# Expert layer in pieces of 64 rows: two experts per step on the two column halves of TensorE

## The reference

```
logits = einsum('bsd,de->bse', x, w_gate)
local_gate = sigmoid(x @ w_local)
for b, for s:
    fresh_e = argmax(logits[b, s])
    e = fresh_e if s == 0 or local_gate[b, s] < 0.5 else prev_e
    prev_e = e
    p = softmax(logits[b, s])
    h = maximum(x[b, s] @ w1[e], 0)
    out[b, s] = p[e] * (h @ w2[e])
```

## Time and profile before

| | |
|---|---|
| median of 3 runs | 992.5 us (991.58 to 993.65) |
| the profiled execution | 993.9 us, of it 992.2 us span |
| TensorE matmuls busy | 947.2 us (95%) |
| TensorE weight loads busy | 732.5 us (74%) |
| VectorE busy | 465.9 us (47%) |
| ScalarE busy | 270.5 us (27%) |
| GpSimd busy | 275.8 us (28%) |
| first matmul of the expert stage | 686.3 us |

### The profile page before, as it was taken

The page is one execution under the profiler, slowest core; times in us unless marked ns, Lnnn a source line. Parts: engine busy times, 40 slices in busy tenths (PEclk is TensorE's granted clock), DMA queues, the critical chain, the costliest instruction groups (busy, mean ns, idle before and its releaser), DMA issues.

```text
span 992.2 us, 51897 instructions
## 1 busy us (share of the span) xinstructions
PE 947.2 (95%) x23581; PEld 732.5 (74%) x23582; DVE 465.9 (47%) x964; ACT 270.5 (27%) x503; POOL 275.8 (28%) x297
## 2 busy tenths in 40 slices
PE   4689999999999999999999999999999999999995
PEld 3579989899898996454554554557888888888884
DVE  5447877887887762423143143162352322222220
ACT  1224444444444442201202202202212122122120
POOL 4535566556656651000011010010052101111111
PEclk9789999999999999999999999999999999999999
DMA  5216442333333321780100100047421111001000
GB/s 147 64 50 209 140 123 89 114 104 119 96 115 111 89 72 41 238 271 0 38 27 24 42 28 20 1 133 256 130 88 61 34 34 39 23 28 33 27 29 3
DMA packets 57704, 81.63 MB, mean 82 GB/s; under 512 B 22274, under 2 KB 37454, under 8 KB 57648
## 3 DMA queue, kind: packets, MB, share of 16 engines
q1 hardware_dynamic: 33536, 58.87, 19.0%
q10 hardware_dynamic: 21088, 13.32, 5.2%
q0 software_dynamic: 3024, 8.72, 2.4%
HBM read 68.04 MB, written 14.45 MB: 83 GB/s over the span
## 4 chain that ended last, share of the span: by engine, by line
PE 91%; issue 3%; DVE 2%; DMA 2%; POOL 1%; ACTq 0%; ACT 0%; POOLq 0%; SPq 0%; DVEq 0%
PE ps_D L1478 14%; PE ps_D L224 12%; PE ps_G L1460 6%; PE ps_E L1460 6%; PE ps_B L236 5%; PE ps_E L956 5%; PE ps_B L188 3%; PE ps_G L1467 3%; PE ps_D L1039 3%; PE ps_A L930 3%; PE ps_G L188 3%; PE ps_D L990 2%; PE ps_E L954 2%; PE ps_E L188 2%; PE ps_D L930 2%
## 5 line engine op out<-in xcount | busy, mean ns | idle before, releaser
L1478 PE MATMUL ps_D<-room,hT 128*128 x496 | 139.1, 433 | 0.8 <-issue 0.8
L224 PE MATMUL ps_D<-room 128*128 128x384 f32 x384 | 126.7, 489 | 0.6 <-DVE room L291 0.6
L1478 PEld LDWEIGHTS ps_D<-room,hT 128*128 128x128 f32 x496 | 91.8, 190 | 35.9 <-issue 1.3
L224 PEld LDWEIGHTS ps_D<-room 128*128 128x128 f32 x384 | 72.1, 190 | 51.5 <-issue 1.6
L1421 POOL DMA_INDIRECT out<-y,token x31 | 35.6, 1147 | 258.3 <-DVE y L1585 224.7
L550 POOL DMA_INDIRECT sorted_rows<-rows,slot x24 | 23.9, 997 | 278.3 <-DVE slot L542 272.2
L894 POOL TENSOR_TENSOR room<-room 32x256 f32<-32x256 f32 x96 | 69.5, 724 | 106.5 <-DVE room L1310 101.1
L1521 ACT ACTIVATE hT<-ps_G 128x512 f32<-128x512 f32 x31 | 18.5, 598 | 217.6 <-PE ps_E L1467 211.4
L1585 DVE TENSOR_SCALAR y<-ps_D,x_in 128x320 f32<-128x320 f32 x31 | 17.0, 550 | 125.9 <-PE ps_D L1478 117.5
L1568 DVE COPY w_own<-room 128x1024 f32 x62 | 44.9, 729 | 62.3 <-PE ps_G L1460 33.8
L291 DVE TENSOR_TENSOR room<-ps_D,room 128x384 f32<-128x384 f32 x32 | 17.8, 558 | 113.2 <-PE ps_D L224 107.8
(11 more groups left out here) (225 smaller groups left out, 1646.2 us busy)
## 6 DMA issues: line engine op xcount, KB each, us to landing
room<-in_moe_w SPq DMA_DIRECT2D x8, 1280.0 KB, 12.6
room<-in_moe_w SPq DMA_DIRECT2D x8, 1024.0 KB, 9.2
room<-in_kb SPq DMA_DIRECT2D x48, 160.0 KB
room<-in_vt SPq DMA_DIRECT2D x24, 320.0 KB, 3.1
x_in<-sorted_rows ACTq DMA_DIRECT2D x27, 161.0 KB, 2.3
room<-in_w SPq DMA_DIRECT2D x48, 82.7 KB
room<-in_a SPq DMA_DIRECT2D x48, 80.0 KB
room<-in_r SPq DMA_DIRECT2D x48, 80.0 KB
```

Source lines behind the costliest of these rows:

```text
L224: mm = pe.matmul(self.vs_bank[n % 2][:, 0:TH], self.v[:, s, d * P:(d + 1) * P], self.wspT[:, s, t * TH:(t + 1) * TH], start=(s == 0), stop ...
L1478: mm = pe.matmul(self.ps_y, side.hT[:, u % 2, f, :], self.weights.w2[:, bass.ds(e, 1), f, :], start=(f == 0), stop=(f == self.NF - 1))
```

## The change

Rows are sorted into pieces of 64 rows; each expert's region is rounded up to 64 in place of 128. 3072 rows are 48 pieces, the rounding needs up to 7 more, and 55 pieces make 28 steps of two pieces. The tables hold pieces. Each piece of a step has its own expert. `fetch` loads two pieces of 64 rows to the two halves of `x_in`. `hidden` computes the first 64 tokens with the first expert's w1, then the other 64 with the second's; every weight block of 128 columns is split into two of 64, whose outputs lie in the lower and upper half of the partitions, that is on the two column halves of the array. `project` does the two pieces on the two column halves as well, the first with w2 in place, the second with a copy of its expert's w2, which ScalarE makes per step (`fetch_w2`). VectorE's `fetch_w1` runs twice per step. In turn t it now copies the second half of step t+1 and the first half of step t+2. After the waits of each group of matmuls TensorE increments a semaphore (`passed`) that nobody waits for. The SBUF room for DMA descriptors is cut to 4096 bytes a partition to make place for `w2_own` (8 x 320 floats).

The diff, cut to its core:

```
-SORTED_TILES = ALL_TILES + EXPERTS - 1
+SORTED_HALVES = TOKENS // HALF + EXPERTS - 1
+STEPS = (SORTED_HALVES + 1) // 2
...
-CAP = ALL_TILES
+CAP = TOKENS // HALF
...
-NT = 32
+NT = 2 * STEPS
...
+        self.w2_own = sb("w2_own", E_FF // P, DM)
...
-        self.table(dve, c, upto[:, :], weight[:, :], 0, FIRST, None, self.first_known)
+        self.table(dve, c, upto[:, :], weight[:, :], 0, 2 * FIRST, None, self.first_known)
...
-        self.table(dve, c, upto[:, :], weight[:, :], FIRST, SORTED_TILES - FIRST, s.first[:, 0:1], self.all_known)
+        self.table(dve, c, upto[:, :], weight[:, :], 2 * FIRST, NT - 2 * FIRST, s.first[:, 0:1], self.all_known)
...
     def fetch(self, eng, turn, u):
+        for h in range(2):
+            at = eng.value_load(self.side.tile_at[0:1, bass.ds((turn * self.SLOTS + u) * 2 + h, 1)], min_val=0,
+                                max_val=BLANK_HALF)
+            eng.dma_start(self.side.x_in[h * HALF:(h + 1) * HALF, u, :],
+                          self.by_half[bass.ds(at, 1), :, :].rearrange("o p n -> (o p) n")).then_inc(self.s_in[u], 16)
...
     def hidden(self, pe, turn, u):
 
         side, t = self.side, turn * self.SLOTS + u
-        x = side.xTt[:, u % 2]
         pe.wait_ge(self.xt_out, self.FREE + t + 1)
...
+        for h in range(2):
+            tokens = slice(h * HALF, (h + 1) * HALF)
+            x = side.xTt[:, u % 2, :, tokens]
+            for half in range(2):
+                pe.wait_ge(self.w1_in, self.parts_done(t, h, half))
+                if h == 0:
+                    pe.wait_ge(self.h_out, self.FREE + 2 * t + half - 1)
+                pe.sem_inc(self.passed, 1)
+                for f in range(4):
+                    for k in range(NK - 1):
+                        for c in range(2):
+                            lo = (half * 4 + f) * P + c * HALF
+                            mm = pe.matmul(self.ps_h[half][c * HALF:(c + 1) * HALF, f, tokens],
+                                           side.w1_own[:, k, lo:lo + HALF], x[:, k, :],
+                                           start=(h == 0 and f == 0 and k == 0), stop=False, skip_group_check=True)
+                mm.then_inc(self.h_made, 1)
+            pe.wait_ge(self.w1_in, self.parts_done(t, h, 2))
+            pe.sem_inc(self.passed, 1)
             for f in range(4):
...
+                for half in range(2):
+                    kept = slice(half * self.REST, (half + 1) * self.REST)
+                    for c in range(2):
+                        lo = f * P + c * HALF
+                        mm = pe.matmul(self.ps_h[half][c * HALF:(c + 1) * HALF, f, tokens],
+                                       side.w1_rest_own[kept, lo:lo + HALF], x[kept, NK - 1, :],
+                                       start=False, stop=True, skip_group_check=True)
             mm.then_inc(self.h_made, 1)
...
+        pe.wait_ge(self.w2_in, t + 1)
         pe.wait_ge(self.y_out, self.FREE + t)
         pe.wait_ge(self.h_out, self.FREE + 2 * t + 2)
+        pe.sem_inc(self.passed, 1)
+        first, second = slice(0, HALF), slice(HALF, P)
         for f in range(self.NF):
-            mm = pe.matmul(self.ps_y, side.hT[:, u % 2, f, :], self.weights.w2[:, bass.ds(e, 1), f, :],
+            pe.matmul(self.ps_y[first, :], side.hT[:, u % 2, f, first], self.weights.w2[:, bass.ds(e, 1), f, :],
+                      start=(f == 0), stop=(f == self.NF - 1))
+            mm = pe.matmul(self.ps_y[second, :], side.hT[:, u % 2, f, second], side.w2_own[:, f, :],
                            start=(f == 0), stop=(f == self.NF - 1))
...
+    def fetch_w2(self, act, turn, u):
+
+        side, w2, t = self.side, self.weights, turn * self.SLOTS + u
+        e = act.value_load(side.tile_expert[0:1, bass.ds(2 * t + 1, 1)], min_val=0, max_val=self.E - 1)
+        w2.until_loaded(act, e)
+        if not isinstance(turn, int) or t >= 1:
+            act.wait_ge(self.y_made, t)
+        act.activation(side.w2_own[:, :, :], w2.w2[:, bass.ds(e, 1), :, :].rearrange("p o f n -> p (o f) n"),
+                       ACT.Copy).then_inc(self.w2_in, 1)
+
     def tile_act(self, act, turn, u):
         t = turn * self.SLOTS + u
+        self.fetch_w2(act, turn, u)
...
     def tile_dve(self, dve, turn, u):
         side, t = self.side, turn * self.SLOTS + u
+        if self.has(turn, u, 1):
+            self.fetch_w1(dve, *self.at(turn, u, 1), 1)
         if self.has(turn, u, 2):
-            self.fetch_w1(dve, *self.at(turn, u, 2))
-        dve.wait_ge(self.s_in[u], 16 * (turn + 1))
+            self.fetch_w1(dve, *self.at(turn, u, 2), 0)
+        dve.wait_ge(self.s_in[u], 32 * (turn + 1))
...
         dve.wait_ge(routing.first_known, 1)
-        self.fetch_w1(dve, 0, 0)
+        self.fetch_w1(dve, 0, 0, 0)
         routing.choose(dve, self.LAST)
-        self.fetch_w1(dve, 0, 1)
+        self.fetch_w1(dve, 0, 0, 1)
+        self.fetch_w1(dve, 0, 1, 0)
         routing.scan(dve, self.LAST)
...
-    nc = bacc.Bacc("TRN2", target_bir_lowering=False, num_devices=1)
+    nc = bacc.Bacc("TRN2", target_bir_lowering=False, num_devices=1, dynamic_dma_scratch_size=4096)
```

More of the change, by code:

```diff
@@ L555, in later @@
         sb = Carver(c.wide, 0, 2 * SEQ)
-        return (sb("over", EXPERTS, CAP), sb("past", NT, EXPERTS), sb("weighed", NT, EXPERTS), sb("te", NT),
-                sb("at", NT), sb("count", EXPERTS), sb("tiles", EXPERTS), sb("upto", EXPERTS), sb("weight", EXPERTS),
+        later = NT - 2 * FIRST
+        return (sb("over", EXPERTS, CAP), sb("past", later, EXPERTS), sb("weighed", later, EXPERTS), sb("te", later),
+                sb("at", later), sb("count", EXPERTS), sb("tiles", EXPERTS), sb("upto", EXPERTS), sb("weight", EXPERTS),
                 sb("need", EXPERTS), sb("blank", PAY))
@@ L597, in first_tiles @@
         dve.wait_ge(self.back, 16 * (BATCH - 1))
-        link(dve, dve.tensor_scalar(count[:, :], s.base[:, :], -float(P - 1), None, ALU.add))
+        link(dve, dve.tensor_scalar(count[:, :], s.base[:, :], -float(HALF - 1), None, ALU.add))
         link(dve, dve.tensor_tensor(count[:, :], count[:, :], s.region[:, :], ALU.subtract))
@@ L1348 @@
 class Experts:
-    E, S = EXPERTS, SORTED_TILES
+    E, S = EXPERTS, STEPS
     NF = E_FF // P
@@ L1414, in sync @@
         weights.load(sp, EXPERTS - 1)
-        routing.fill_blank_tile(sp)
+        routing.fill_blank_half(sp)
     def put(self, pool, turn, u):
@@ L1447, in turn_x, with parts_done @@
         mm.then_inc(self.xt_made, 1)
+    def parts_done(self, t, h, part):
+        return 6 * t + 3 * h + part + 1
     def hidden(self, pe, turn, u):
         side, t = self.side, turn * self.SLOTS + u
-        x = side.xTt[:, u % 2]
         pe.wait_ge(self.xt_out, self.FREE + t + 1)
-        for half in range(2):
-            pe.wait_ge(self.w1_in, 3 * t + half + 1)
-            pe.wait_ge(self.h_out, self.FREE + 2 * t + half - 1)
-            for f in range(4):
-                col = (half * 4 + f) * P
-                for k in range(NK - 1):
-                    mm = pe.matmul(self.ps_h[half][:, f, :], side.w1_own[:, k, col:col + P], x[:, k, :],
-                                   start=(f == 0 and k == 0), stop=False, skip_group_check=True)
-            mm.then_inc(self.h_made, 1)
@@ L1463, in hidden @@
-        pe.wait_ge(self.w1_in, 3 * t + 3)
-        for f in range(4):
-            for half in range(2):
-                kept = slice(half * self.REST, (half + 1) * self.REST)
-                mm = pe.matmul(self.ps_h[half][:, f, :], side.w1_rest_own[kept, f * P:(f + 1) * P], x[kept, NK - 1, :],
-                               start=False, stop=True, skip_group_check=True)
-        mm.then_inc(self.h_made, 1)
+        for h in range(2):
[16 more added lines that the diff above has]
+            pe.sem_inc(self.passed, 1)
+            for f in range(4):
+                for half in range(2):
[5 more added lines that the diff above has]
+                                       start=False, stop=True, skip_group_check=True)
+            mm.then_inc(self.h_made, 1)
@@ L1541, in scalar @@
                 self.turned_x(act, 0, i - 3)
+        act.wait_ge(routing.first_known, 1)
         self.relu(act, 0, 0)
@@ L1548, in scalar @@
         routing.copy_expert(act, self.LAST)
-        act.wait_ge(routing.first_known, 1)
         self.peeled(act, self.tile_act, 2, 3)
@@ L1556, in scalar, with fetch_w1 @@
         self.every_tile(act, self.tile_act)
-    def fetch_w1(self, dve, turn, u):
+    def fetch_w1(self, dve, turn, u, h):
         side, w1, t = self.side, self.weights, turn * self.SLOTS + u
-        e = dve.value_load(side.tile_expert[0:1, bass.ds(t, 1)], min_val=0, max_val=self.E - 1)
+        e = dve.value_load(side.tile_expert[0:1, bass.ds(2 * t + h, 1)], min_val=0, max_val=self.E - 1)
         w1.until_loaded(dve, e)
-        later = not isinstance(turn, int) or t >= 1
+        later = not isinstance(turn, int) or t >= 1 or h >= 1
         for half in range(2):
```

47 lines of the change are left out of this document (23 added, 24 removed).

## The result

The changed kernel took 1022.1 us (median; 1019.3 to 1026.8), the kernel before 993.1 in the same measurement: a ratio of 1.030, 95% interval 1.027 to 1.033. Slower, as forecast (1014.9, range 997 to 1032), and 7 us above the forecast time. The profiled execution took 1020.3 us, its span is 1018.6.

What follows compares the result with a forecast made beforehand. TensorE was taken to bound the expert stage at full clock. Three steps fewer -28 us, the other steps +26, the last +2, the entry +22: forecast 1014.9 us, range 997 to 1032.

Steps and rivals of the forecast that it cites:

- Steady step: Expert stage: hidden layer, remainder, transposes, projection and shape changes make a step of 10.45 us, against 9.45 before.
- eight changes of shape: TensorE in each step: new boundaries between matmul groups of different array shape, eight at 0.15, cost 1.2 us.
- Entry: Start of the expert stage: second halves fetched a turn later, behind the last batch's routing; +22 us in all.
- Term (a): Entry, first_tiles: twice the compared elements and a longer table, between two gates TensorE awaits; +0.75 us.
- (d): Entry, after projections 1 to 3: weigh, place, other_tiles delay second-half copies; stalls 0.85, 1.3, 6.8, plus 1.9 low clock.
- Last step: Between the last two projections nothing covers the w2 copy: 2.5 + 0.5 replace a 0.8 gap, +2 us.
- Code: Unrolled steps: TensorE stalls 0.3 us for instructions about every other step; +2 us.
- rival B: Expert loop's code does not stay: two returns cost 4 us each, dense blocks stall again; 1025 us, chance 0.18.
- stops without partner in the unrolled steps: Expected sign: TensorE halting mid-group with no engine releasing it, from code arriving late, 0.3 us each.
- A (cheap boundaries): Expert step: boundary 0.05, round 0.054 give a step of 9.36 and 986.6 us; faster or same, chance 0.12.
- C: Column halves run one after the other: step 18.4 us, time about 1220 us; chance 0.04.
- D: Entry: split_rows transfers land sooner, 3 us instead of 6.3; idle 3.4, 4 us less, 1010; no separate chance given.

Runs made afterwards that it cites:

- e5_again: Changed kernel with w1 copies ahead of routing, loop written out, earlier register load, no w2 copy for the blank last piece; chip B: 987.4 us, ratio 0.9956.
- e4: Changed kernel with TensorE's register load of the expert's number moved ahead of the hidden layer; chip A: 1035.3 us, ratio 1.043.
- e2: Changed kernel with all five second-half w1 copies moved ahead of the routing's work; measured twice on chip A: 1032.9 and 1029.4 us.
- e1: Changed kernel with only the second half's w1 copy of step 1 moved ahead of scan; chip A: 1043.2 us, ratio 1.050.
- e6: Changed kernel with the second column half's matmuls left out of the first layer; chip A: 1013.9 us, ratio 1.020.
- e7: Changed kernel with whole-width matmuls (128x128 weights, 64 moving columns) in the first layer in place of column-half pairs; chip A: 1125.8 us, ratio 1.133.
- e3: Changed kernel with the expert stage's loop, steps 12 to 23, written out; chip A: 1040.3 us, ratio 1.048.
- after_again: The changed kernel unaltered, measured again on chip A: 1045.2 us, ratio 1.052 to the kernel before.
- e5_best: Changed kernel with w1 copies ahead of routing, loop written out, earlier register load, no w2 copy for the blank last piece; chip A: 1011.0 us, ratio 1.018.
- after_third: The changed kernel unaltered, measured a third time, on chip B: 1021.5 us, ratio 1.031 to the kernel before.

## Why the prediction was right, and where it was off

- **Steady step: forecast 10.45, measured 10.43, for partly wrong reasons.** The rounds came at 0.058, not 0.057, the projection at its 4.31. The 1.2 us for eight changes of shape were too much: in e5_again a step is 10.07, and less 3.71 + 0.93 + 0.33 + 4.31 that leaves 0.79, or 0.10 each. The rest, 0.36, is the load of the expert's number (0.30 on A, by e4), which my sum did not have. It is in the trace of before at most as part of a small gap, and I took that for a change of shape.
- **Entry: forecast first projection 708.9, measured 709.15; stalls forecast 6.7, 0.85, 1.3 and 6.8, measured 6.35, 0.75, 1.41 and 6.60.** The stalls are the best-founded part: the order of VectorE's list, and the durations of its rows. That the first projection agrees to 0.3 us is partly luck. The terms written down for it add up to 710.2, not 708.9, and the roundings that are to make up 1.3 are not given. Term (a) expected the first hidden layer 0.75 us later; it began 1.3 earlier (685.06 against 686.34 before). A stop of 1.56 us for code at 693.34, which is in no term, took most of that back. And by the figures of (d) the stall after place would be 1.6 (3.4 + 0.7 - 2.5), not 1.3. The granted clock was 0.50 in the idle time, 0.65 from 758 to 762 and 1.00 after; from projection 3 to projection 4 it is 18.65 us, 8.2 more than a step, forecast 8.7. e2 undoes these stalls and gets back 12 to 16 of them on A. What I did not see is that two of them lay over waits for code. The first, 1.31, with the 1.56 behind it, becomes a single stop of 2.88 when the copy is moved (e5_again), so nothing is won there; of the second, 6.35, there remain 2.94 in e1 and 1.18 in e5_again.
- **Last step:** the w2 copy of 2.34 us ends late; 3.2 us idle, 7.7 from projection to projection, forecast 7.3. But only 10.5 us follow the last projection's start, where I had taken over the 13.8 of before. The last write is issued 6.0 us after that start in both kernels (984.46, and 1014.07); the span then goes on for 7.7 us before and 4.5 after, and why is not known. On B the same program has 12.2 us behind that start. There the last projection, after 3.11 us of idle time, ran at a granted clock of 0.58 (1008 to 1012 us), where it had 1.00 in the first measurement after 3.20; its write is issued 7.7 us after the start, and again 4.5 follow.
- **Code: forecast 2 in the unrolled steps and nothing in the loop; measured none in the unrolled steps but the 1.56 us at 693.34, and 5.3 at the loop's two returns.** They cost 2.3 and 3.0 us (12.94 and 13.66 against loop steps of 10.68). This is rival B, which had 4 each and a chance of 0.18. Its effect came, and so did its cause: the body of 1.95 thousand instructions is loaded anew and those of 1.2 thousand are not (e6, e7), and written out (e3) the returns' cost is gone. The ten other loop steps are 0.25 longer than unrolled ones: that is the register load again (e4 brings 11.27 to 10.70 and the unrolled 10.97 to 10.67), not code, and another 2.5. Together 7.8 in the loop. The stops without partner in the unrolled steps, which the prediction named as a sign, came on A alone, and there they go with GpSimd's scatters.
- **The sum:** span 1018.6 against 1014.6. First projection +0.2; from there to the last projection but one 291.2 against 284.6, +6.6, of which the loop's 7.8 and -1.2 for the rest (the 2 us for code that didn't come there, -0.5 from 25 steps at 10.43, and some 1.3 of small differences); the last +0.4; the tail -3.3. Makes +4. The failed term is the loop, and that the sum is off by only 4 is luck: the tail, taken over from the kernel before, gave back 3.3 of it. It was luck as well which chip measured: on A the same kernel takes 1045.2, outside the range, by the stops that no term has.
- **Rivals.** A (cheap boundaries) would have needed a step of 9.6. With boundaries of 0.10 its mechanism is half right, but the step stays at 10.07 when everything else is taken away, and the hidden layers of two pieces take 3.71 us where one tile of 128 rows took 3.57. B came true, within the main case's range of times. C fell with e6. D did not come: scan starts at 701.17 after 6.99 us of waiting, as long as before.

So the steps alone favour the change: 28 of 10.07 are 282 us, 31 of 9.45 are 293. What made it 3% slower was mostly not its arithmetic but a second half whose weights came one turn later, a register load 28 times on the path, and loop returns; e5 on B, 0.44% faster than the kernel before, shows it. On A the same four edits leave it 1.8% slower.

## What to carry to other kernels

Count what is on the path ahead of each long group, register loads too, and don't book an unexplained gap as the nearest thing with a name. When a resource is wanted a turn earlier than before, go through the list of the engine that fills it and move the fill ahead of every unrelated job; here that was 12 to 16 us. Count the instructions of a loop's body, and look at the instruction queue while the loop repeats: packets there mean that every return may stop the engine. Before a dense stream of small instructions is called good, measure it on more than one chip: this one differed by 24 us where its predecessor differed by 2, and single edits looked like losses of 1 to 2% until the unaltered kernel ran beside them.

## What the runs showed of the hardware

- With 64 moving columns, a matmul of 128x128 weights takes 0.112 us and one of 128x64 takes 0.058; with 128 moving columns the first takes 0.112 as well. Two column halves run at once at no cost to each other (16 or 32 matmuls in 0.93 us).
- A change of sub-array shape cost about 0.10 us on average in e5_again, counted with the waits beside it.
- A loop body of 1.2 thousand TensorE instructions (e6, e7), and the first stage's of 1.7 thousand, repeat without instruction packets; one of 1.95 thousand is loaded in each round (24 packets from 846 to 970 us against 4), and its returns cost 2.3 and 3.0 us. At the entry of the stage TensorE stands 0.9 to 3 us for code on both chips and goes on 1.3 to 1.5 us after the packet has landed. The Trainium skill (Runtime: NRT & Kernel Launch, Instruction fetch mechanics) calls such crossings mostly hidden, which held for the unrolled steps on B and not at the entry. It also says that a branch to code not held stalls; the returns of 2.3 and 3.0 us agree.
- On chip A a dense stream of 128x64 matmuls stood about 0.3 us in nearly every step, each time 0.7 to 0.9 us after the start of a scatter by GpSimd (18 stops in after_again, 20 in e5_best); on chip B the same program with the scatter at the same place never did.
- A stage of dense matmuls after 6 to 7 us of idle time ran its first 32 of them in 1.98 instead of 1.15 us, at a granted clock of 0.50. After 3.1 to 3.2 us of idle time the clock was 0.58 in one run (after_third) and 1.00 in another.
